# Two pairs of short tasks set between the last long ones of the last MLP, in an attention, MLP and routed-expert kernel

## The reference

```python
# 1. attention: 4 batches x 8 heads, 576 x 64
scores = where(scale*q@k.T >= rowmax - tau, scale*q@k.T, -1e9)
x = softmax(scores) @ v                      # -> (4, 576, 512)
# 2. MLP
u = x + (xt @ U @ V).transpose(0, 2, 1)      # token mixing, rank 32
x = u + relu(u @ w_ch1) @ w_ch2              # 512 -> 2048 -> 512
# 3. routed experts: each row goes to one of 8 experts
logits = x @ w_gate; gate = sigmoid(x @ w_local)
e = argmax(logits[s]) if s == 0 or gate[s] < 0.5 else previous e
out[s] = softmax(logits[s])[e] * (relu(x[s] @ w1[e]) @ w2[e])
```

## Time and profile before

| what | value |
|---|---|
| median of 3 runs | 1110.26 us (1107.96 to 1113.25) |
| profiled execution | 1106.8 us, of it span 1105.1 us |
| TensorE matmul (PE) busy | 1053.1 us, 95% |
| DVE, ACT, POOL busy | 514.0, 469.6, 371.2 us |
| last long task of the last MLP ends | 801.14 us into the span |
| both halves' `gates` written | 804.01 us |
| first expert tile's product begins | 836.88 us |

### The profile page before, as it was taken

How to read it: one execution, slowest core, us unless ns; L and a number is a source line. 1 busy time by engine, 2 the same in 40 slices (tenths; PEclk the granted TensorE clock), 3 DMA queues, 4 the chain that set the end, 5 groups by cost and what they waited for, 6 DMA issues and landing times.

```text
span 1105.1 us, 20107 instructions
## 1 busy us (share of the span) xinstructions
PE 1053.1 (95%) x7142; PEld 923.2 (84%) x7143; DVE 514.0 (47%) x1022; ACT 469.6 (42%) x914; POOL 371.2 (34%) x341
## 2 busy tenths in 40 slices
PE   6999899999989999998999999999988999999996
PEld 5665799999779999977998997999977788888885
DVE  4675554445454444544444452322275534245641
ACT  5675543444454443455434343322114433244530
POOL 4454322623502462451146224079411112111121
PEclk9999999999999999999999999999999999999998
DMA  7887151525352452525143213232065533154611
GB/s 160 189 183 187 39 125 55 140 88 130 102 120 55 123 140 84 134 78 143 23 135 103 86 47 115 101 134 77 1 218 188 164 127 128 50 197 161 212 34 41
DMA packets 110730, 127.54 MB, mean 115 GB/s; under 512 B 67229, under 2 KB 67229, under 8 KB 110624
## 3 DMA queue, kind: packets, MB, share of 16 engines
q1 hardware_dynamic: 104480, 114.54, 36.5%
q0 software_dynamic: 3600, 11.01, 3.1%
q10 hardware_dynamic: 2544, 0.59, 0.2%
HBM read 88.16 MB, written 10.22 MB: 89 GB/s over the span
## 4 chain that ended last, share of the span: by engine, by line
PE 82%; SPq 6%; ACT 3%; DVE 3%; issue 3%; DMA 2%; POOL 0%; ACTq 0%; DVEq 0%; POOLq 0%
PE mlp_banks L697 19%; PE mlp_banks L689 18%; PE p_down L1387 11%; PE p_up L1387 10%; PE aux L647 6%; PE score_banks L623 5%; PE score_banks L630 5%; PE p_turn L1414 2%; DMA mlp_rows<-z_rows 1%; PE aux L590 1%; PE p_x L1381 1%; SPq L291 1%; PE mlp_banks L672 1%; DVE stat L939 1%; PE mlp_banks L679 1%
## 5 line engine op out<-in xcount | busy, mean ns | idle before, releaser
L794 ACT ACTIVATE ex<-score_banks,stat 128x576 f32<-128x576 f32 x132 | 97.7, 740 | 178.1 <-DVE stat L939 178.0
L469 POOL CAST w_hi<-stage 128x1024 fp32r<-128x1024 f32 x64 | 66.5, 1039 | 288.2 <-PE mlp_banks L689 240.2
L697 PE MATMUL mlp_banks<-hid_hi,w_hi 128*128 128x320 f32 (+1 forms) x512 | 158.7, 310 | 0.8 <-DVE hid_lo L987 0.8
L689 PE MATMUL mlp_banks<-u_hi,w_hi 128*128 128x320 f32 (+1 forms) x512 | 157.2, 307 | 2.1 <-ACT u_hi L843 1.7
L948 DVE SCALAR_TENSOR_TENSOR ex<-score_banks,stat,ex 128x576 f32<-128x576 f32 x132 | 107.7, 816 | 107.4 <-ACT stat L798 105.6
L474 POOL TENSOR_TENSOR w_lo<-stage,w_hi 128x1024 fp32r<-128x1024 f32 (+1 forms) x70 | 154.0, 2201 | 4.8
L697 PE MATMUL mlp_banks<-hid_lo,w_hi 128*128 128x320 f32 (+1 forms) x512 | 151.5, 296 | 0.0
L697 PE MATMUL mlp_banks<-hid_hi,w_lo 128*128 128x320 f32 (+1 forms) x512 | 151.5, 296 | 0.0
L689 PE MATMUL mlp_banks<-u_hi,w_lo 128*128 128x320 f32 (+1 forms) x512 | 151.5, 296 | 0.0
L689 PE MATMUL mlp_banks<-u_lo,w_hi 128*128 128x320 f32 (+1 forms) x512 | 151.4, 296 | 0.0
L987 DVE SCALAR_TENSOR_TENSOR hid_lo<-mlp_banks,hid_hi 128x256 fp32r<-128x256 f32 (+1 forms) x128 | 58.4, 456 | 113.1 <-ACT hid_hi L845 112.5
(11 more groups left out here) (238 smaller groups left out, 1819.1 us busy)
## 6 DMA issues: line engine op xcount, KB each, us to landing
stage<-in_moe_w_ch SPq DMA_DIRECT2D x64, 512.0 KB, 3.7
w_raw<-in_moe_w SPq DMA_DIRECT2D x64, 512.0 KB, 5.1
q_tiles<-q_parts SPq DMA_DIRECT2D x30, 320.0 KB, 3.9
q_tiles<-q_parts SPq DMA_DIRECT2D x60, 160.0 KB, 4.1
k_tiles<-k_parts SPq DMA_DIRECT2D x60, 144.0 KB, 3.4
raw_q<-in_q SPq DMA_DIRECT2D x32, 128.0 KB, 3.1
raw_v<-in_v SPq DMA_DIRECT2D x32, 128.0 KB, 3.0
raw_k<-in_k SPq DMA_DIRECT2D x28, 128.0 KB, 2.7
```

Of the source, the lines that this page charges most:

```text
L469: nc.gpsimd.tensor_copy(w_hi[:, n % RING], stage[:, n % 2]).then_inc(w_upper, 1)
L689: last = nc.tensor.matmul(bank[:, 0:w], ch1(a, g, d, c), of[:, d, cols], start=(d == 0 and n == 0), stop=(d == KC - 1 and n == 2))
L697: last = nc.tensor.matmul(bank[:, 0:w], ch2(a, g, q, c), of[:, q, 0:w], start=(q == 0 and n == 0), stop=(q == QUARTER - 1 and n == 2))
L794: nc.scalar.activation(ex_of(n), score_of(n), ACT.Exp, bias=stat[:, n % 4, 0:1], scale=-1.0).then_inc(exp_done, 1)
```

## The change

Only the last batch's list is changed. What stood behind its last `channel` task was gate 0, gate 1, logits 0, logits 1, rows 0, rows 1, rows 2. Now gate 0 and rows 0 stand between the second and the third `hidden` task of the second half's last quarter, logits 0 and rows 1 between its second and third `channel` task, and behind the last `channel` task come gate 1, rows 2 and logits 1. Nothing is added to or left out of the work; the waits of lines 664 and 665 now look at other neighbours, and the bank of each task follows its new place.

```diff
-        tasks += [(b, "gate", k, 0, 0) for k in range(2)]
-        tasks += [(b, "logits", k, 0, 0) for k in range(2)]
-        tasks += rows[:SPLIT_ROWS]
+        if b < B - 1:
+            tasks += [(b, "gate", k, 0, 0) for k in range(2)]
+            tasks += [(b, "logits", k, 0, 0) for k in range(2)]
+            tasks += rows[:SPLIT_ROWS]
+        else:
+            tasks[-6:-6] = [(b, "gate", 0, 0, 0), rows[0]]
+            tasks[-2:-2] = [(b, "logits", 0, 0, 0), rows[1]]
+            tasks += [(b, "gate", 1, 0, 0)] + rows[2:SPLIT_ROWS] + [(b, "logits", 1, 0, 0)]
         waiting = rows[SPLIT_ROWS:]
     return tasks + waiting
```

## The result

The changed kernel takes 1112.6 us (median of 20 runs, 1109.3 to 1114.5) where the kernel before, in 20 runs, takes 1107.8 us. The ratio is 1.0037 (95% interval 1.0027 to 1.0047): slower by 0.37%, some 4.1 us (3.0 to 5.2). The medians lie 4.8 us apart and the means 4.4. The forecast was 1113.3 us and 3.0 us more; "same" by its bound of 0.5%. The kernel before had been given with 1110.26 us from three runs, so that the forecast's absolute number came out within 0.7 us is luck: that base was 2.5 us high. What has to be judged is the difference, 3.0 for 4.1.

What follows compares the result with a forecast made beforehand. TensorE, busy 95% of the span, was taken to bound the kernel. The pairs' 1.78 + 1.31 = 3.09 us, less 0 to 0.1, gave 3.0 us on the 1110.3 us median: 1113.3 us, range 1109.5 to 1116.7.

Steps and rivals of the forecast that it cites:

- "same" by its bound of 0.5%: Whole kernel: a difference within about 0.5% (5.6 us) can't be told from no change; chance of this outcome 0.84.
- TensorE has no hole in the last quarter, so what is put there is paid.: Last quarter of the last MLP: TensorE busy 15.00 of 15 us in 786 to 801, so moved tasks lengthen the kernel.
- First pair 1.78 us, second 1.31 us.: Gate 0 with rows 0 between hidden tasks costs 1.78 us; logits 0 with rows 1 between channel tasks 1.31 us.
- The waits of 0.6 and 0.5 us: TensorE waits for DVE to leave a bank ahead of rows 0, about 0.6 us, and rows 1, about 0.5 us.
- The end gives nothing back.: Behind the last channel task, the chain to DVE's reduce of logits 1 stays 2.5 us; gain 0, at most 0.1 us.
- the 0.1 us kept as a possible gain: Gate 1 might start at most 0.10 us earlier without gate 0 ahead of it; taken as 0, kept for the range.
- The row blocks held nothing up, so their leaving gains nothing.: Routing behind logits 1: the keep transposes also need POOL's plane and the choices, so earlier row blocks gain 0.
- The transpose's price by the row and not by the figure of the Trainium skill: Moved transposes: 0.12 us each by the profile row; the skill's 275 ns would make the sum about 4.6 us.
- rival B: Full round trips in the pairs, or one clock fall in 804 to 806: 4.3 or 3.0 + 1.7 us; chance 0.14.
- Rival C, the clock falling in the long tasks.: First pair to last channel task: one clock fall there, one after logits 1, 6.4 us more, 1116.7 us; chance 0.05.
- The sign that the forecast named, 1.00 from 786 to 836: The changed kernel's profile shows a granted clock of 1.00 from 786 to 836 us if the forecast holds.

Runs made afterwards that it cites:

- own_banks: The change with gate 0, rows 0, logits 0 and rows 1 writing two PSUM banks of their own: 1110.8 us, ratio 1.0014 to the kernel before.
- singles: The change with its four moved tasks each alone between long tasks instead of in pairs: 1114.43 us, ratio 1.0055 to the kernel before.
- rows2_behind: The change with rows 2 behind logits 1 instead of ahead of it: 1110.54 us, ratio 1.0019 to the kernel before.
- one_pair: The kernel before with only rows 0 and rows 1 moved, between the second and third channel task: 1109.6 us, ratio 1.0013.
- after_all_filled: The change with 21 identity transposes in the first expert tile and 13 between logits 1 and the keep transposes: 1107.05 us, ratio 0.9990 to the kernel before.
- before_filled: The kernel before with 21 identity transposes where TensorE waits in the first expert tile: 1103.47 us, ratio 0.9962.
- gate_split_filled: before_filled with gate 1's first three products issued ahead of the wait for the last add: 1103.92 us, ratio 0.9966 to the kernel before.
- before_shifted: The kernel before with 21 identity transposes at the very start, where TensorE waits for q: 1103.99 us, ratio 0.9972.
- the shifted pair, The pair at the start: The kernel before and the change, each with 21 identity transposes at the very start: 1103.99 us and 1108.67 us.
- the filled kernels: Kernels with 21 identity transposes where TensorE waits in the first expert tile: medians from 1103.47 to 1107.05 us.
- the filled pair: The kernel before and the change, each with 21 identity transposes in the first expert tile: 1103.47 us and 1106.48 us.
- delay_only: The kernel before with 26 identity transposes behind the second hidden task of the last quarter's second half, old task order: 1106.97 us, ratio 0.9995.

## Why the prediction was right, and what it missed

*TensorE has no hole in the last quarter, so what is put there is paid.* Right: the stretch grew by 3.07 us.

*First pair 1.78 us, second 1.31 us.* Right within 0.02: DVE's hid_lo of the third hidden task follows that of the second after 3.53 us (790.65 to 794.18) where a long task takes 1.76, so 1.77; the add of the third channel task follows that of the second after 3.06 us (798.99 to 802.05), so 1.30. The waits of 0.6 and 0.5 us are in the waits of TensorE, and own_banks and singles show that they are for banks.

*The end gives nothing back.* Right: 2.50 for 2.51 us, and rows2_behind shows rows 2 to be free in its new place. Gate 1 started 0.14 us after the add without gate 0 ahead of it, so that 0.15 us was the wake, and the 0.1 us kept as a possible gain does not show.

*The row blocks held nothing up, so their leaving gains nothing.* Right, by one_pair and by the unchanged distance behind.

*The transpose's price by the row and not by the figure of the Trainium skill ("TensorE: Matmul & The Clock Gate", Part 4: PE-mode transpose).* Right: own_banks pays 1.81 us for the four tasks where the row gave 1.8.

*Against 3.0 us, 4.1 were measured.* The interval of the 4.1 reaches down to 3.0, so some of the difference may be scatter. The term that was too small is most likely the clock's, which the forecast set at 0 and kept under rival B (0.14). B's place was not borne out: it put the fall where the row blocks had stood, and after_all_filled shows no gain from filling that hole. The profiled fall stood at the second expert tile, behind waits that the change doesn't touch.

Two things speak for the clock. One is the profiles, between 800 and 850: all ten kernels with a longer stretch show one or two falls there, 3.4 to 10.2 us at 0.50 in all, and of the four with the stretch as before (before, before_filled, gate_split_filled, before_shifted) only the last shows one, of 3.4 us; and where both of a pair have one fall, the shifted pair, nothing is left beside the stretch. That is one execution of each. The other is the clock of all executions: over the 24 of the kernel before that ran beside the filled kernels, the time is longer by 0.6 us for each 0.001 less of mean granted clock (correlation 0.68). The change had 0.9921 and the kernel before, in those 24, 0.9935, which is 0.8 us, and 3.07 + 0.8 is 3.9 for 4.1 by the ratio and 4.4 by means. The pair at the start gives 3.07 + 0.6 x 2.2 = 4.4 for 4.0 by means, the filled pair 3.07 + 0.3 = 3.4 for 3.7, and there the two clocks are not apart beyond their scatter. This is a correlation, argued and not shown: no pair of kernels was compared at the full clock throughout. Why a longer stretch should bring falls in the routing and the first tiles stays open. In delay_only's one profile a shift by 2.8 us, without the new order, stands with a fall at 826.3 and none at the second tile, so it need not be the holes of the new order.

*Rival C, the clock falling in the long tasks.* Wrong: 1.00 in 786 to 804 of the change and in 786 to 810 of singles, which has twice the waits. The sign that the forecast named, 1.00 from 786 to 836, holds in the changed kernel's one profile, where the fall comes at 838.6; in own_banks and delay_only it comes before 836. What the Trainium skill ("TensorE: Matmul & The Clock Gate", A second HAM failure mode: psum-queue depth-cycling) reports of short idles between groups of matmuls found no support there; the two falls shown, at 514 and at the second tile, came when TensorE had been busy 0.72 and 0.57 of 2 us.

## What to carry to other kernels

A short task that fills a wait is free where it stands, and a chain with holes in it is no evidence that its members cost anything; ask what the array would do in that time without them before moving them into a stretch that is full. With two banks in turn, a short task between long ones also costs the emptying of the long one ahead of it, so short ones go in pairs, or better, by the trace (13.66 us for 14.92), into banks of their own. And compare variants of a kernel only after looking at the last product for a wait on nothing: twenty idle instructions were worth as much as the change.

## What the runs showed of the hardware that was not expected

- Adding 21 to 34 transposes to TensorE's program, at the start, in the MLP or in the first tile, took a gap of 1.84 us out of the last product, in all eight kernels that have them; the six without show gaps of 1.48 to 2.02 us. From its first matmul to its last end the product takes 9.5 us before (1088.69 to 1098.22) and 5.9 us in before_filled. Only a part of this is the gap. The other part is the fallen clock, and that doesn't always follow the gap: in one_pair's profile 1.85 us of gap are followed by a clock of 1.00 and by 5.16 us for the rest of the product, where it was 6.71. The added transposes gave 0.28% (before_shifted) to 0.38% (before_filled, where the fillers stand in waits too), as much as the change lost.
- 2.83 us of additional work on the engine that bounds the kernel cost nothing in the median (delay_only), most likely for that reason: its last product takes 5.8 us.
- Executions of the kernel before differ by up to 8.5 us (1104.8 to 1113.25), and those with less granted clock are on the whole the longer ones. One fall of 6.8 us, from 838.6 on, cost 2.7 us at the second tile, where TensorE waited through a part of it.
- before_filled, with the highest mean clock of all kernels (0.9970), also scattered least: 1101.9 to 1104.2 us in seven executions.
